# Moving two score shifts, two key sums and the row-sum inversion by one or two steps on VectorE

## The reference: what is computed

```python
kv_flat = kv_pool.reshape(B, -1, C) @ w_sr        # 768 keys of 128 features; k = v = kv_flat
s = scale * (q @ k.transpose(0, 2, 1))
s = s - s.max(-1, keepdims=True)
a = np.exp(s)
a /= a.sum(-1, keepdims=True) + 1e-09
x = a @ v                                         # 12288 tokens of 128 features

h = x @ w_in                                      # 2048 wide
g = np.where(pos, h, np.where(neg, 0.0, (h + 1) ** 2 / 4))   # pos: h >= 1, neg: h <= -1
x = g @ w_out
h = x @ w_in2
g = h * (1.0 / (1.0 + np.exp(-1.702 * h)))
out = g @ w_out2
```

## Time and profile before

| | |
|---|---|
| median of 3 runs | 1349.87 us (1349.83 to 1350.0) |
| profiled execution: time, span | 1349.87 us, 1348.0 us |
| PE busy | 1285.1 us, 95% of the span |
| PEld busy | 1037.2 us, 77% |
| DVE busy | 1073.4 us, 80% |
| ACT busy | 1022.2 us, 76% |
| POOL busy | 1007.3 us, 75% |
| mean granted TensorE clock | 0.987 |

### The profile page before, as it was taken

One profiled execution on the slowest core, in us unless ns is written; L12 is line 12 of the kernel. 1 busy time (PEld: TensorE's weight loads), 2 busy tenths in 40 slices (PEclk: granted clock), 3 DMA queues, 4 the chain that ended last, 5 costly groups with the idle time before them and its releaser, 6 DMA issues.

```text
span 1348.0 us, 17128 instructions
## 1 busy us (share of the span) xinstructions
PE 1285.1 (95%) x5496; PEld 1037.2 (77%) x5496; DVE 1073.4 (80%) x1235; ACT 1022.2 (76%) x1083; POOL 1007.3 (75%) x411
## 2 busy tenths in 40 slices
PE   4558999999999999999999999999999999999988
PEld 3346788888888888888888888888888888887866
DVE  6899887887887888888878878878888888776433
ACT  3655787878778788788878787787887888796756
POOL 1636797797797887977977977978879779779770
PEclk9878999999999999999999999999999999999999
DMA  9100000000000000000000000001000000000000
GB/s 337 40 16 16 9 32 17 16 22 25 16 16 16 31 16 16 31 16 16 31 16 16 25 22 16 16 16 31 16 16 31 16 16 24 9 17 16 0 9 16
DMA packets 18605, 36.19 MB, mean 27 GB/s; under 512 B 3344, under 2 KB 3472, under 8 KB 18320
## 3 DMA queue, kind: packets, MB, share of 16 engines
q1 hardware_dynamic: 18576, 35.83, 8.3%
HBM read 29.43 MB, written 6.39 MB: 27 GB/s over the span
## 4 chain that ended last, share of the span: by engine, by line
PE 90%; DVE 4%; DMA 2%; issue 1%; POOL 1%; ACT 1%; SPq 0%; DVEq 0%; POOLq 0%; ACTq 0%
PE ps_ring L344 17%; PE ps_ring L346 17%; PE ps_ring L345 17%; PE ps_y L344 13%; PE ps_y L346 13%; PE ps_y L345 13%; DMA kv_sb<-in_kv_t 1%; DVE pt_lo L641 1%; POOL g_lo L314 1%; DVE g L760 1%; DVE s_sb L703 1%; DMA key_max<-max_row 0%; DVE part_sum L709 0%; DVE g_hi L753 0%; SPq L232 0%
## 5 line engine op out<-in xcount | busy, mean ns | idle before, releaser
L314 POOL TENSOR_TENSOR g_lo<-g,g_hi 128x1024 fp32r<-128x1024 f32 x192 | 525.2, 2735 | 122.6 <-DVE g L760 101.8
L307 POOL TENSOR_TENSOR g_lo<-g,g_hi 128x1024 fp32r<-128x1024 f32 x181 | 437.0, 2414 | 146.2 <-ACT g_hi L573 146.2
L571 ACT ACTIVATE g<-ps_ring 128x1024 f32<-128x1024 f32 x192 | 197.1, 1027 | 186.6 <-PE ps_ring L346 186.3
L753 DVE SCALAR_TENSOR_TENSOR g_hi<-g,ps_ring 128x1024 fp32r<-128x1024 f32 x192 | 234.0, 1219 | 130.1 <-ACT g L587 128.3
L344 PE MATMUL ps_y<-g_hi,w_hi 128*128 128x512 f32 x768 | 307.0, 400 | 14.9 <-POOL g_lo L314 12.4
L346 PE MATMUL ps_y<-g_hi,w_lo 128*128 128x512 f32 x768 | 303.6, 395 | 0.0
L345 PE MATMUL ps_y<-g_lo,w_hi 128*128 128x512 f32 x768 | 300.7, 392 | 0.0
L760 DVE SCALAR_TENSOR_TENSOR g<-g,ps_ring 128x1024 f32<-128x1024 f32 x192 | 233.0, 1213 | 0.0
L580 ACT ACTIVATE g<-ps_ring 128x1024 f32<-128x1024 f32 x192 | 197.9, 1030 | 14.5 <-POOL g_lo L314 8.5
L587 ACT ACTIVATE g<-g 128x1024 f32<-128x1024 f32 x192 | 203.7, 1061 | 5.4
L573 ACT ACTIVATE g_hi<-ps_ring 128x1024 fp32r<-128x1024 f32 x192 | 196.1, 1021 | 5.4 <-PE ps_y L346 5.4
(11 more groups left out here) (70 smaller groups left out, 1731.5 us busy)
## 6 DMA issues: line engine op xcount, KB each, us to landing
kv_sb<-in_kv_t SPq DMA_DIRECT2D x12, 512.0 KB, 8.5
q_sb<-in_q_t SPq DMA_DIRECT2D x24, 256.0 KB, 3.7
key_max<-max_row SPq DMA_DIRECT2D x24, 256.0 KB, 3.4
inv_sum<-inv_row SPq DMA_DIRECT2D x24, 256.0 KB, 3.2
out_t<-y_sb SPq DMA_DIRECT2D x24, 256.0 KB, 3.4
w_raw<-in_moe_w_in SPq DMA_DIRECT2D x2, 1024.0 KB, 17.0
max_row<-max_turned SPq DMA_DIRECT2D x24, 2.0 KB, 1.3
inv_row<-inv_turned SPq DMA_DIRECT2D x24, 2.0 KB, 1.3
```

Source lines behind the costliest of these rows:

```text
L307: nc.gpsimd.tensor_tensor(g2_lo[:, slot, :], g2[:, slot, :], g2_hi[:, slot, :].bitcast(F32), ALU.subtract).then_inc(g2_lo_done, 1)
L314: nc.gpsimd.tensor_tensor(g1_lo[:, slot, :], g1[:, slot, :], g1_hi[:, slot, :].bitcast(F32), ALU.subtract).then_inc(g1_lo_done, 1)
L571: nc.scalar.activation(g2[:, slot, :], ps_h2(k), ACT.Gelu_apprx_sigmoid).then_inc(g2_done, 1)
L753: nc.vector.scalar_tensor_tensor(out=g1_hi[:, uu % 2, :], in0=g1[:, uu % 2, :], scalar=1.0, in1=ps_h1(k), op0=ALU.min, op1=ALU.max).then_i ...
```

## The change

Three things are edited, all on VectorE, and all but the last of them in the steps of iterations 3 and later:

- `shift` of the second pair of chunks moves from step 5 to step 6, that of the third pair from step 6 to step 7.
- `add_keys` of the second pair moves from step 3 to step 5, that of the third from step 4 to step 5; `invert` moves from step 5 to step 6.
- The addition of 1e-9 to the 32 x 16 row sums takes the number as an immediate (`tensor_scalar`) instead of a second operand `eps` in SBUF. The buffer `eps` and the memset that fills it go away. This one is in `invert`, so it holds for all 24 tiles.

```diff
-        eps = sb(ctx, "eps", [SQ, QB])
...
-            nc.vector.memset(eps[:, :], 1e-9).then_inc(rows_cleared, 1)
...
-                nc.vector.tensor_tensor(row, row, eps[:, :], ALU.add).then_inc(eps_added, 1)
+                nc.vector.tensor_scalar(row, row, 1e-9, None, ALU.add).then_inc(eps_added, 1)
...
                     if k == 4:
                         shift(it, half, 0)
-                    if k == 5:
+                    if k == 6:
                         shift(it, half, 1)
-                    if k == 6:
+                    if k == 7:
                         shift(it, half, 2)
                 if is_tile(it - 1):
                     if k == 3:
                         add_keys(it - 1, 1 - half, 0)
+                    if k == 5:
                         add_keys(it - 1, 1 - half, 1)
-                    if k == 4:
                         add_keys(it - 1, 1 - half, 2)
-                    if k == 5:
+                    if k == 6:
                         invert(it - 1)
...
-            dve.wait_ge(rows_cleared, 3)
+            dve.wait_ge(rows_cleared, 2)
```

## The result

The changed kernel takes 1369.31 us (median of 4 runs, 1368.35 to 1370.78) against 1349.93 us for the kernel before: ratio 1.0142 with a 95% interval of 1.0125 to 1.0160, 19.4 us slower. The forecast was 1377.5 us. The wait that it named is there, once per iteration. But something else, not named in it, gave back 8 us.

The account below looks back on a forecast made before the run. TensorE was taken to bound the kernel; 27.4 + 1.1 - 0.9 = 27.6 us on 1349.87 us gave 1377.5 us, 2.0% slower. The forecast of 1370 to 1384 us had 0.65; the range was 1361 to 1389 us.

Parts of the forecast that it names:

- The bound: In iterations 4 to 22 TensorE sets the pace, busy 1048.00 of 1048.00 us, so any new wait is paid in full.
- the slack of 1.5 us: VectorE's copy of chunk 0 is out at about 672.1, 1.5 us before TensorE's score chunk 2 at 673.60.
- the place: Head of the next block, where score chunk 2 needs VectorE's copy of chunk 0: 1.37 us lost per iteration.
- The price of a held shift: A shift issued while GpSimd subtracts waits for its end, then runs about 1.07 us: 2.31 us in all against 1.22.
- the chain of steps 5 to 7: Held shifts in steps 6 and 7 start the copy of chunk 0 at 674.13, making score chunk 2 1.27 us late.
- The three terms of the sum: 27.4 us for iterations 3 to 22, plus 1.1 behind iteration 23, less 0.9 won in iteration 3: 27.6 us.
- The addition: VectorE's eps addition in the inversion: 1.16 us if it waits for GpSimd, 0.16 if not; left open.
- low 2 of step 7: One of GpSimd's two subtractions in step 7, put at 670.70 to 673.06, holding up the third shift.
- A: Rival: third shift not caught, costs 1.22 us; 1364 us with half the wait (0.12), 1349 to 1350 without (0.07).
- B: Rival: more than one wait, or the shift's upper bound: 1.8 us or more, 21 times, 1388 us; chance 0.12.
- C: Rival: faster, as GpSimd gains, the addition is free and the copy is out before 673.60: 1346.7 us; chance 0.04.
- low 1 of step 3: One of GpSimd's two subtractions in step 3; the prediction names such a pair per step, with no size for this one.

Follow-up runs that it names:

- the moves alone: Five moved calls as in the change, but buffer eps, its memset and the tensor_tensor addition kept, against the kernel before: 1376.80 us, ratio 1.0201.

## Why the prediction was right in the change of order, and where it was not

- **The bound, the slack of 1.5 us, the place.** Right: all 19 named waits of the steady part are for the copy of chunk 0.
- **The price of a held shift and the chain of steps 5 to 7.** Right, shown by the moves alone: copies at 3.95 us behind the block's start against 3.93, 1.42 us per iteration against 1.37, 1376.8 us against 1377.5. The three terms of the sum can be read from the block starts of that trace. From block 4 to block 24 it loses 28.75 us (1077.28 against 1048.53) where 27.4 was forecast. Iteration 3 gives back 0.96 where 0.9 was: its blocks 3 and 4 start at 92.56 and 145.30, before at 92.23 and 145.93. Iteration 24 costs 0.54 us (49.89 against 49.35) where 1.1 was: the late start of its step 0 costs some 0.9, but its later waits are shorter. The profiled executions differ by 28.7 us and the medians by 27.5, so the agreement with 27.6 to 0.1 us is in part luck.
- **The addition.** I left open whether it waits; it does (1.15 us). By the prediction's sum this makes no difference, since low 2 of step 7 covers the shift either way; no run has the addition free there.
- **Rivals.** A (the shift isn't caught) is what happens in every second iteration when the third shift is moved alone, but not here. By its time alone the result would look like it: 1369.3 lies between A's 1364 us and the forecast, 0.7 us below the 1370 to 1384 that had 0.65. B: no second wait. C: its 1346.7 us needed the moves to be free, and they weren't.
- **What failed: the removal of the buffer `eps` had no term in the sum**, and TensorE's pace was taken as fixed. Removing 64 bytes moved the buffers behind them, and a step fell from 5.53 to 5.44 us. That is worth 12 us with the old order (1337.25 against 1349.33). With the new order it is worth 7.5 to 8 (1369.3 against 1376.8 and 1377.3): TensorE gains some 0.67 us per iteration in the steps, but the wait grows from 1.42 to 1.79 us. A reading of the traces, not tested apart: GpSimd's row of subtractions from low 1 of step 3 to low 2 of step 7 has no gaps and keeps its pace, 19.80 us from start to start (659.64 to 679.44) against 19.83 with the moves alone (664.88 to 684.71), so the 0.36 us that TensorE gains in the last four steps come back as waiting. The profiled executions of the changed kernel and the kernel before differ by 18.5 us: 22.6 lost from block 4 to block 24 and 0.2 in iteration 24, less 0.9 up to block 3, 2.3 in iteration 3 and 1.2 behind iteration 24.

So the total of 19.4 us against 27.6 is the mechanism at about its forecast size less an effect that the forecast lacked.

## What to carry to other kernels

TensorE had no gaps here, and the slack that counted was the 1.5 us ahead of one copy. An instruction put in front of such a slack is to be priced as it runs there, under a neighbour that can hold it up, not as its fastest row. A test of an edit that adds or removes a buffer needs a twin in which the bytes stay allocated: here 64 unused bytes per partition made 12 us with the old order, a little under half of what the reordering costs. The version to keep is the one with the old order and the immediate addition, 1337.25 us.

## What the runs showed of the hardware that was not expected

- The pace of back-to-back 128x512 matmuls depends on where buffers lie: 0.2267 us from start to start in the steps of one layout, 0.228 to 0.233 in those of all others, at a granted clock of 1.00, and also for matmuls whose own operands hadn't moved.
- A two-input VectorE instruction that waits for GpSimd usually gets in when GpSimd's instruction ends (held up for 0.5 to 2.2 us in the rows above), but it can be passed over at two ends in a row: 6.45 us for a 1.2 us subtraction, in four iterations of one trace. TensorE then lost 3.3 us in the iteration, and the kernel's time spread over 20 us from run to run.
- 0.06 us in the order of issue decided between 1.22 and 3.43 us, and it alternated from iteration to iteration.
